# Attention and two expert blocks on one core: the last stage's first loads in other buffers and earlier, sums ahead of splits, loads behind the first two stores

## What is computed

```python
# q, k, v: 8 x 8 x 576 x 64;  x: 4608 x 512 after it
scores = q @ k^T / 8;  x = (scores * decay[head]) @ v        # decay: lower triangle, gamma^distance
h = maximum(maximum(x @ w1, x @ w2), x @ w3)                 # 4608 x 768
x = h @ w_out                                                # 4608 x 512
a = x @ u1;  b = x @ u2;  h = (a * b) @ u3                   # 4608 x 1024
out = h @ u_out                                              # 4608 x 512
```

## Time and profile before

| | us |
|---|---|
| median of 3 runs | 1333.28 (1332.85 to 1336.16) |
| profiled execution | 1333.16 |
| its span | 1331.4 |
| PE busy | 1259.7 (95%) |
| DVE busy | 803.4 (60%) |
| ACT busy | 459.7 (35%) |
| POOL busy | 452.3 (34%) |

### The profile page before, as it was taken

One profiled execution on the slowest core, in us unless ns is written; L12 is line 12 of the kernel. 1 busy time (PEld: TensorE's weight loads), 2 busy tenths in 40 slices (PEclk: granted clock), 3 DMA queues, 4 the chain that ended last, 5 costly groups with the idle time before them and its releaser, 6 DMA issues.

```text
span 1331.4 us, 20535 instructions
## 1 busy us (share of the span) xinstructions
PE 1259.7 (95%) x8032; PEld 1235.0 (93%) x8032; DVE 803.4 (60%) x1194; ACT 459.7 (35%) x707; POOL 452.3 (34%) x248
## 2 busy tenths in 40 slices
PE   6999878999999999999999999999999998499999
PEld 5888867999999999999899999999999997499999
DVE  5555668656455555548889677454535537756762
ACT  2112112433333232325455444232323323344442
POOL 2333566602020202006598562202012007635550
PEclk8999988999999999999999999999999999799999
DMA  8778786302020202031655541313313133334441
GB/s 312 235 239 288 252 286 223 133 29 95 25 95 31 89 31 90 31 137 54 224 180 176 174 157 53 109 48 101 104 58 102 52 130 120 130 137 148 155 142 66
DMA packets 82929, 174.37 MB, mean 131 GB/s; under 512 B 8976, under 2 KB 57488, under 8 KB 82832
## 3 DMA queue, kind: packets, MB, share of 16 engines
q1 hardware_dynamic: 82832, 173.05, 37.9%
HBM read 109.58 MB, written 63.44 MB: 130 GB/s over the span
## 4 chain that ended last, share of the span: by engine, by line
PE 74%; DMA 10%; DVE 9%; issue 4%; POOL 1%; SPq 1%; ACT 1%; DVEq 0%; POOLq 0%
PE ps L944 23%; PE ps L945 23%; PE ps L946 23%; DVE clo L699 3%; DMA vks<-vk 3%; DMA u3raw<-u3T 2%; DVE wlo L699 2%; DMA x2d<-h 2%; DMA gd<-h 1%; PE ps L890 1%; PE ps L875 1%; PE ps L900 1%; DVE state L728 1%; DVE probs L709 1%; POOL qdec L499 1%
## 5 line engine op out<-in xcount | busy, mean ns | idle before, releaser
L944 PE MATMUL ps<-chi,whi 128*128 128x384 f32 x2016 | 678.7, 337 | 32.4 <-DVE wlo L699 15.3
L945 PE MATMUL ps<-clo,whi 128*128 128x384 f32 x2016 | 676.4, 336 | 0.0
L946 PE MATMUL ps<-chi,wlo 128*128 128x384 f32 x2016 | 676.3, 335 | 0.0
L499 POOL TENSOR_TENSOR raw<-raw,raw 128x768 f32<-128x768 f32 (+2 forms) x96 | 273.3, 2866 | 536.7 <-DMA raw<-xd 222.0
L944 PEld LDWEIGHTS ps<-chi,whi 128*128 128x128 f32 x2016 | 380.7, 189 | 37.9 <-issue 18.6
L945 PEld LDWEIGHTS ps<-clo,whi 128*128 128x128 f32 x2016 | 380.9, 189 | 0.0
L946 PEld LDWEIGHTS ps<-chi,wlo 128*128 128x128 f32 x2016 | 380.7, 189 | 0.0
L699 DVE TENSOR_TENSOR clo<-raw,chi 128x768 fp32r<-128x768 f32 (+2 forms) x168 | 259.5, 1567 | 16.5 <-ACT chi L622 16.1
L622 ACT CAST chi<-raw 128x768 fp32r<-128x768 f32 (+2 forms) x168 | 180.7, 1081 | 93.8 <-PE ps L946 86.6
L689 ACT COPY w<-ps 128x384 f32<-128x384 f32 x126 | 60.8, 482 | 253.7 <-PE ps L946 252.2
L675 ACT COPY u<-ps 128x384 f32<-128x384 f32 x126 | 60.8, 482 | 168.1 <-PE ps L946 166.6
(11 more groups left out here) (41 smaller groups left out, 917.1 us busy)
## 6 DMA issues: line engine op xcount, KB each, us to landing
qks<-qk SPq DMA_DIRECT2D x32, 576.0 KB, 4.4
vks<-vk SPq DMA_DIRECT2D x32, 576.0 KB, 6.0
gd<-h SPq DMA_DIRECT2D x96, 192.0 KB, 1.9
raw<-gd SPq DMA_DIRECT2D x24, 768.0 KB, 7.2
hd<-h SPq DMA_DIRECT2D x72, 192.0 KB, 1.9
raw<-hd SPq DMA_DIRECT2D x24, 576.0 KB, 5.7
raw<-xd SPq DMA_DIRECT2D x24, 384.0 KB, 5.4
x2d<-h SPq DMA_DIRECT2D x48, 192.0 KB, 2.5
```

The source lines that it names most:

```text
L499: return nc.gpsimd.tensor_tensor(out_, a, b, op)
L944: nc.tensor.matmul(to, w1, x1, start=(start and k == 0), stop=False, skip_group_check=True)
L945: nc.tensor.matmul(to, w1, x2, start=False, stop=False, skip_group_check=True)
L946: last = nc.tensor.matmul(to, w2, x1, start=False, stop=(k == KH[st] - 1), skip_group_check=True)
```

## The change

There are four edits.

1. **Stage O's buffers lie elsewhere.** The raw blocks 0, 3 and 2 of O go where stage I has its own raw blocks, block 6 to a place that I doesn't use, the others to weights' places that come free early; weight set 19 goes to the place of sets 11 and 12, which are read for the last time by P3 of unit 107. The four loads of O's first tile are issued in iteration 107 (110 before), set 19 in 109 (110, at its end, before); POOL's adds for the tile stand in 109 and 110 (112 and 113), for set 19 in 110 (111), its splits in 111 (112).
2. **One buffer for position 6.** In C and O position 6 has one buffer in place of two.
3. **Loads in two parts.** For the second to sixth tile of C and O, SP issues blocks 0, 3 and 2 behind the stores of H11 and H10, and block 6 at the end of the iteration, when all seven positions of the tile before are split.
4. **Sums ahead of splits.** On DVE, position 3 is split behind `sum22`, 4 behind the next sum and so on, position 6 last; position 1 moves ahead of `sum11`.

The diff, cut to its core (the tables for the change from C to I and two lines of `SLOT_FREE` are left out):

```diff
-HI_IO = {("end", "s"): [0], ("end", "u"): [1], ("end", "p2"): [2], ("next", "p5"): [3],
-         ("next", "p3"): [4, 5, 6]}
-LO_STD = {("end", "21"): [0], ("end", "11"): [1, 2], ("next", "start"): [3], ("next", "22"): [4],
-          ("next", "21"): [5], ("next", "12"): [6]}
...
+HI_IO = {("end", "s"): [0], ("end", "u"): [1], ("end", "p3"): [2], ("end", "p2"): [3],
+         ("next", "p5"): [4], ("next", "p3"): [5, 6]}
+LO_STD = {("end", "21"): [0], ("end", "12"): [1], ("end", "11"): [2], ("next", "22"): [3],
+          ("next", "21"): [4], ("next", "12"): [5], ("next", "11"): [6]}
...
+LO_IO = {("end", "21"): [0], ("end", "12"): [1], ("end", "11"): [2, 3], ("next", "22"): [4],
+         ("next", "11"): [5, 6]}
...
-          19: ((109, P3), 18), 20: ((111, P3), 0)}
+          19: ((107, P3), 0), 20: ((110, P3), 18)}
...
-             18: 69, 20: 112}
+             18: 69, 19: 109, 20: 112}
...
-            17: 69, 18: 70, 19: 111, 20: 113}
+            17: 69, 18: 70, 19: 110, 20: 113}
...
-        _a = {C: 48, I: None, O: 110}[_st]
-        T_AT[_tau] = {C: (50, 51), I: (65, 65), O: (112, 113)}[_st]
+        _a = {C: 48, I: None, O: 107}[_st]
+        T_AT[_tau] = {C: (50, 51), I: (65, 65), O: (109, 110)}[_st]
...
-        raw_base = [0, 0, 0, 144384]
-        comb_base = [150528, 79872, 79872, 57344]
+        raw_at = [[i * KH[st] * N * 4 for i in range(7)] for st in range(3)]
+        raw_at.append([0, 173056, 12288, 6144, 137216, 179200, 187392])
+        comb_base = [150528, 79872, 79872, 47104]
...
-                  + [28672 * n for n in range(2)])
+                  + [144384, 18432])
...
-            if pos == 6 and st in (C, O) and tau % 2:
-                return raw[st][7]
-            return raw[st][pos]
+            return raw[tau // TILES][pos]
...
                 if t == 0:
+                    if st != B:
+                        sp.wait_ge(c_lo, 7 * tau)
...
-                for pos, j, k in ((0, 0, 0), (3, 1, 0), (6, 1, 1), (2, 0, 1)):
-                    sp.dma_start(raw_block(tau, pos)[:, :, :], acts[st][2 * t + j, k, :, :, :]
-                                 ).then_inc(raw_loaded[LOADED[pos]], 16)
+                for pos in (0, 3, 6, 2):
+                    if pos != 6 or t == 0 or st in (B, I):
+                        load_raw_block(tau, pos)
+
+            def load_raw_rest(tau):
+                sp.wait_ge(c_lo, 7 * tau)
+                load_raw_block(tau, 6)
...
-                if it in RAW_AT:
-                    load_raw(RAW_AT[it])
+                tau = RAW_AT.get(it)
+                two_parts = tau is not None and tau // TILES in (C, O) and tau % TILES
+                if tau is not None and not two_parts:
+                    load_raw(tau)
...
                         store(g, 1, 1)
                         sp.wait_ge(copied21, COPIED[g])
                         store(g, 1, 0)
+                        if two_parts:
+                            load_raw(tau)
                         sp.wait_ge(sum12, g + 1)
                         store(g, 0, 1)
...
-                if it == 110:
-                    load_weight(19)
+                if two_parts:
+                    load_raw_rest(tau)
...
+                    elif tau == O * TILES:
+                        pool.wait_ge(prod, DONE[(108, P3)])
                     add(x(1), x(6), x(4), ALU.subtract).then_inc(combined, 1)
```

More of the change, by code:

```diff
@@ L103 @@
          ("next", "p4"): [5], ("next", "p3"): [6]}
-HI_IO = {("end", "s"): [0], ("end", "u"): [1], ("end", "p2"): [2], ("next", "p5"): [3],
-         ("next", "p3"): [4, 5, 6]}
-LO_STD = {("end", "21"): [0], ("end", "11"): [1, 2], ("next", "start"): [3], ("next", "22"): [4],
-          ("next", "21"): [5], ("next", "12"): [6]}
-LO_CI = {("end", "12"): [0], ("next", "start"): [1, 2], ("next", "22"): [3, 4], ("next", "21"): [5],
-         ("next", "12"): [6]}
-LO_IO = {("end", "21"): [0], ("end", "11"): [1, 2], ("next", "22"): [3], ("next", "12"): [4, 5],
-         ("next", "11"): [6]}
+HI_IO = {("end", "s"): [0], ("end", "u"): [1], ("end", "p3"): [2], ("end", "p2"): [3],
+         ("next", "p5"): [4], ("next", "p3"): [5, 6]}
+LO_STD = {("end", "21"): [0], ("end", "12"): [1], ("end", "11"): [2], ("next", "22"): [3],
+          ("next", "21"): [4], ("next", "12"): [5], ("next", "11"): [6]}
+LO_CI = {("end", "12"): [0], ("next", "start"): [1], ("next", "22"): [2, 3], ("next", "21"): [4],
+         ("next", "12"): [5], ("next", "11"): [6]}
+LO_IO = {("end", "21"): [0], ("end", "12"): [1], ("end", "11"): [2, 3], ("next", "22"): [4],
+         ("next", "11"): [5, 6]}
 def due(std, ci, io, it, point):
@@ L199, in build @@
             kh = KH[st]
-            blocks = 8 if st in (C, O) else 7
-            raw.append([at(f"raw{st}_{i}", [P, kh, N], f32, raw_base[st] + i * kh * N * 4)
-                        for i in range(blocks)])
+            raw.append([at(f"raw{st}_{i}", [P, kh, N], f32, raw_at[st][i]) for i in range(7)])
             size = 2 * kh * N * 4
@@ L385, in load_weight, with load_raw_block @@
                 sp.dma_start(w21[wi][:, :, :], src[:, 3, :, :]).then_inc(w_loaded[wi % 3], 16)
+            def load_raw_block(tau, pos):
+                st, t = divmod(tau, TILES)
+                j, k = {0: (0, 0), 3: (1, 0), 6: (1, 1), 2: (0, 1)}[pos]
+                sp.dma_start(raw_block(tau, pos)[:, :, :], acts[st][2 * t + j, k, :, :, :]
+                             ).then_inc(raw_loaded[LOADED[pos]], 16)
             def load_raw(tau):
```

20 lines of the change are left out of this document (4 added, 16 removed).

## The result

| | before | changed |
|---|---|---|
| median, us | 1334.72 (4 runs, 1332.85 to 1337.61) | 1318.96 (4 runs, 1315.87 to 1320.51) |
| ratio to before | | 0.9877, 95% interval 0.985 to 0.9905 |
| span of the profiled execution | 1331.4 | 1317.7 |

The account below looks back on a forecast made before the run. PE, busy 95% of the span, was taken to set the end. From 1333.16 us, minus 17.0 at the change from I to O and plus 5 in stage C gave 1321.2; the 8-in-10 range was 1309 to 1333.

Parts of the forecast that it names:

- Minus 17.0: Change from stage I to O: 63.9 us from the start of iteration 111 to 116, where 80.9 stood.
- plus 5: Stage C: PE loses 12.2 us against 6.6 before; bounds minus 6.6 to plus 21.
- Iterations 111 and 113: End of stage I: early loads free the store, adds finish earlier; minus 3.9 and minus 1.8 us, 7.28 us each.
- The wait at unit 115's P1: Start of stage O: PE waits 4.4 us for wlo20's first half behind seven splits and eight sums or merges.
- The wait before P6: Unit 115: PE waits 8 us for wlo20's second half behind POOL's adds, plus 1.8 us for the clock.
- the ring: Stage C, single buffer: last split through block 6's load to next last split takes 24.2 us, 2.4 over PE's need.
- both signs: Stage C: PE's waits in iterations 54 to 65 sum to about 12 us; block 6 lands within 4 us of issue.
- The port in C: Stage C tiles with weight adds: POOL and DVE alternate, holding the port 23.5 us against PE's 21.8.
- Stage O: Tile to tile in O: ring about 27 us against 29.1 of PE, so no stall, 0 us.
- B (C gains too): Rival: stage C gives minus 2 to minus 6.6 us, whole kernel 1312; chance 0.22.
- C (the wait at unit 115 stays near 10): Rival: early loads only move the wait at unit 115; change of stage gains 8 us, whole kernel 1330; chance 0.15.
- D (block 6 decides everywhere): Rival: block 6 lands in 7.8 us; plus 21 in C, 1342, and O 2 to 3 more per tile; chance 0.13.

Follow-up runs that it names:

- late loads: Changed kernel with stage O's first four loads back in iteration 110 and POOL's adds for them in 112 and 113; 1325.88 us, ratio 0.9914 to before.
- first half moved up too: Changed kernel with both halves of set 20's lo part split together, the first also moved ahead of positions 5 and 6; 1304.79 us, ratio 0.9766 to before.
- small adds: Changed kernel with POOL's four raw adds of tile 19 on 8 columns of each row in place of 384; 1312.64 us, ratio 0.9841 to before.
- two buffers: Changed kernel with two buffers for position 6 in stage C and all four loads there behind the first two stores; 1312.69 us, ratio 0.9849 to before.
- old order: Changed kernel with the old order of sums and splits on DVE (tables STD and CI); 1328.03 us, ratio 0.9945 to before.

## Why the prediction was right, step by step

**The sum.** Minus 17.0 and plus 5 were forecast, minus 15.6 and plus 1.6 came, and 13.7 in the spans against 12. The gain and its place were right; the two errors, 1.4 too much gain and 3.4 too much loss, partly cancel, and that is luck. The plus 1.6 is itself inside the scatter of stage C: it takes 137.0 to 138.6 us in the seven traces with edits 2 to 4 and 137.0 and 138.8 in the two without. So no cost there is shown at all, and plus 5 was at least three times too large.

**Iterations 111 and 113.** Forecast 3.9 and 1.8 us less; all three iterations take 7.3. With the loads late again PE waits 3.2 us in iteration 111, and the whole stretch grows by 9.2 us (late loads). The cover named, the time of stage I, held.

**The wait at unit 115's P1.** Forecast 4.4 us after seven splits and eight sums, ending 37.6 us after the start of 111; it ended after 37.3, and PE waited 3.9. Taking the half out of that list removed wait and clock loss (first half moved up too).

**The wait before P6.** Forecast 8 us, through two POOL adds; 7.7 came. The half was to end 53.8 us after the start of 111, and ended after 54.0. That POOL's adds hold these splits is shown by small adds; that the two alternate, one instruction each, by the 3.54 and 5.50 us in their timelines. What was too small is the clock: 1.8 us for each wait. After the first it took 2.7, after the second 2.9, together 2.0 too much; the two waits were 0.8 shorter than forecast, and some 0.2 went elsewhere. That is the 1.4 us. The size of this term is chance in part: in the second run of the changed kernel the clock took 1.7 and 2.4 us behind the same two waits.

**Stage C.** The step that failed in size is the ring. It was to take 24.2 us and takes 23.3 (last splits ending at 688.06 and 711.40). Up to the end of the four adds, with position 1 split, it is as forecast: 14.9 us, in the sum and in the trace (688.06 to 702.93). But two of its terms were off against each other. Block 6 lands later than the 3.6 us assumed: POOL begins its second add 5.05 us after SP's issue. (The formula that the prediction took from the Trainium skill, DMA: Bandwidth & Descriptors, section "Anatomy of one DMA", is given there for DMAs that GpSimd issues; SP issues this one.)

```profile
688.09 0.32 SPq L386 DMA_DIRECT2D raw<-hd  x1
```

```profile
688.95 2.69 POOL L502 TENSOR_TENSOR raw<-raw,raw 128x1152 f32<-128x1152 f32 x1 [2.10 <-DVE clo L704]
693.14 9.79 POOL L502 TENSOR_TENSOR raw<-raw,raw 128x1152 f32<-128x1152 f32 x3 [1.50 <-DMA raw<-hd]
```

But while POOL waits for it (1.50 us idle ahead of the second line), position 0 goes through beside it; I had put it in turn with the adds. The difference is in the second part of the ring, from there to the last split: 9.3 us forecast, 8.5 in the trace. PE waits 0.8, 1.2 and 1.2 us in iterations 60, 62 and 64, where 2.3, 2.6 and 2.5 were forecast. But a ring of 23.3 us need not be what set these tiles: with two buffers, and so without it, they take 23.1 and 23.0. That it would add anything there is the step that the runs don't bear out. The 3.3 us of iteration 56 (1.1 for ACT's copy, 2.2 for the sum) came as forecast and the clock added 1.7; the 1.1 of iteration 55 did not come, since the add that was to be first began at 641.40, when the split ahead of the sum had begun (640.61). Before, PE waited 2.8 us there. In all PE waits 6.8 us in C where 12 were to be the sign, and block 6 didn't land within 4 us; both signs failed.

**The port in C.** The 23.5 us for tiles with weight adds lie near the 22.7 to 23.2 that came, with the ring and without it. But tiles without weight adds take as long (64 to 66: 23.1 in the changed kernel, 23.0 with two buffers), and moving a weight's adds away made its tile no shorter (23.6). So the agreement is luck. What the tiles from 60 on share is one wait of 0.8 to 1.5 us for the sum ahead of P3; what sets it stays open.

**Stage O.** No stall was forecast after 116, and none came: 155.0 us, as before to a tenth.

**The rivals.** B (C gains too) is out: in none of the seven traces of this code was C shorter than the 137.0 us of the kernel before; even with two buffers it keeps waits of 1.0 to 1.3 us. C (the wait at unit 115 stays near 10) is out as it stands: P1 of unit 115 waits 3.9 us where it waited 10.0. But P6 waits longer, 7.7 in place of 5.6, so that the two still make 11.6 of 15.6 us. D (block 6 decides everywhere) is out: 5 us to land, and no wait in O after 116. With the old order, or with the first half moved up, O does have waits for a sum; that they come through block 6 is not shown.

## What to carry to other kernels

When a stage is prepared early, look at what then stands last in front of its first product: here it was a list in program order, and moving one cast and two subtractions of it gave another 17.0 us there, 14.7 after what stage O gave back, as much as the change. An operation that the critical engine waits for should not stand behind a result which that engine has yet to make. A second buffer that is given up turns its load into a link of a ring; count the ring's time against the period that the stage has anyway, and not against PE's work alone: here it cost on the first full tile and nothing on the later ones. And an agreement of a sum with a time is no proof: change the term and see whether the time follows.
